# The rank product in three strips of the array, and a reordered work list around the batch boundaries of a fused attention and feed-forward kernel

## The chip, the cores and the metric

The kernel runs on one core of a Trainium2 chip. The metric is the device time of one execution in microseconds (us); lower is better. The profile comes from one further execution, whose own time is given below beside its span.

## The reference, cut to what matters

```python
B, H, S, D = 4, 8, 768, 48                     # 4 batches, 8 heads, 768 tokens, head size 48
f = 1 / (1 + exp(-f_logit))
for t in range(S):                             # gated linear attention
    state = f[:, :, t, :, None] * state + einsum('bhd,bhe->bhde', k[:, :, t], v[:, :, t])
    y[:, :, t] = einsum('bhd,bhde->bhe', q[:, :, t], state)
x = y as [B, S, 384]
u = x + ((x^T @ U) @ V)^T                      # token mix of rank 32: U is 768x32, V is 32x768
x2 = u + relu(u @ w_ch1) @ w_ch2               # 384 -> 1536 -> 384
h = relu(x2 @ w_in)                            # 384 -> 1024
c = conv along the tokens, 3 taps per channel
out = (h * sigmoid(c)) @ w_out                 # 1024 -> 384
```

## The kernel before, in words

The program is one list of tasks, `ORDER`, made by `schedule()` (line 69). Every engine walks through the same list and does its own share of each task; between engines there are only semaphores. So a change of the list changes what stands ahead of what on each engine.

**Attention.** A batch has 768 tokens, cut into 3 "duos" of 256 tokens, numbered n = 0 to 11 over the four batches. A duo goes through the steps of `STEPS`: EVEN (-1), levels 0 to 5, T (a transpose), U (state update), Y (outputs). In EVEN VectorE multiplies q by k for the self products (L1019) and q by the gates (L1022), GpSimd multiplies k by the gates (L1163) and then the gates in pairs (L1166). In a level TensorE forms scores with 32 small float32 matmuls in four quadrants of the array, 48 rows by 64 columns each (L585; level 0 has four wider ones ahead of them, L567), and VectorE scales q (L1029, L1040) and takes the scores out of PSUM (L976, L982). Y is L631, and ScalarE copies its result into `x` (L852, L853, L856; the last part of batch 0 on VectorE, L1063). The three duos of batch 0 run at the start with nothing else beside them. Those of batch b+1 run in slots of the feed-forward layers of batch b: `at` maps a slot s to attention steps.

**Layers of a batch.** `rank` forms x^T U: 6 float32 matmuls over the 6 token blocks, 128 rows by 96 columns (U three times side by side) by 384 (L668). ScalarE rounds it into `rstack` (L871) and VectorE writes the rest into rows 64 to 95 (L1070). `mix` transposes x and adds V times rank in the same PSUM bank (L679, L685), and u is split into u_hi and u_lo (ScalarE L876, VectorE L1077). `first1` and `second1` are the first layer pair, 24 slots: each product is made of three float32r matmuls from high and low parts (L700 to L702, L719, L720, L724), nine matmuls a task. `first2` and `second2` are the second pair, 16 slots (L739 to L741, L758, L759, L763). Between them ScalarE does the relu (L905), VectorE the convolution (L1109, L1112 twice), ScalarE the sigmoid (L892), VectorE the product (L1096), ScalarE the rounding (L898) and GpSimd the low part (L1200). `second2` of a task stands three slots after its `first2`. `out` copies three finished PSUM banks to `ostage` (ScalarE, L921).

**Weights.** 44 "pieces" of the weights are loaded during the first slots of batch 0, two per slot: SyncE issues the load, ScalarE rounds the high part (L863), GpSimd subtracts the low part (L1173), through 5 staging buffers.

**PSUM.** The ring `hb` of 3 banks serves rank, mix, first1 and first2 in turn (`ring_free` waits for the user three uses back); `acc` (3 banks) takes second1 and second2, `att` (2 banks) the attention.

**The order at the places in question, before.** Batch 0: Y of duo 1, rank of duo 0, Y of duo 2, rank of duos 1 and 2, pieces, mix 0 to 2, gates of duo 3, then slot 0 (first1, mix 3, EVEN of duo 3), slot 1 (first1, mix 4, 5, level 0 of duo 3), slot 2 (first1, level 1, second1). A batch's end: first2 15, second2 12, rank of the next batch, last2, second2 13, mix 0, mix 1, second2 14, mix 2, second2 15, out.

## Time and profile before

| | |
|---|---|
| median of 3 runs | 736.3 us (735.75 to 736.71) |
| profiled execution, own time | 736.56 us |
| its span, first to last instruction | 734.8 us |
| TensorE matmuls busy | 699.3 us, 95% |
| TensorE weight loads busy | 657.7 us, 90% |
| VectorE busy | 446.1 us, 61% |
| GpSimd busy | 286.3 us, 39% |
| ScalarE busy | 246.3 us, 34% |
| mean granted TensorE clock | 0.993 |

Times in the rows below count from the span's start. A float32 matmul is recorded as two matmul instructions, so the 6 matmuls of a rank are 12 records, and the 32 of an attention level are 64. In a timeline a merged row "x64" gives the start of the first and the time to the end of the last. The end of a matmul is modelled, so distances are read from start to start. The granted-clock column is a share of 2.4 GHz.

### The profile page before, as it was taken

The numbers are of one execution on the slowest core, as the hardware profiler recorded it, in microseconds if no ns is written. First come the engines' busy times: TensorE is split into PE (matmuls) and PEld (weight loads), VectorE is DVE, ScalarE is ACT, GpSimd is POOL, SyncE is SP. The second block draws the span as 40 slices with busy tenths as digits, with TensorE's granted clock in tenths as the row PEclk, the third lists the DMA queues.
The fourth block names the chain that finished last, engine by engine and source line by source line (L and its number), as shares of the span: only waits on it lengthen the run. The fifth ranks groups of instructions, "written<-read, shape, count | busy, mean of one in ns | idle before, by whom it ended". The sixth has DMA issues, their size and how long they took to land.

```text
span 734.8 us, 22489 instructions
## 1 busy us (share of the span) xinstructions
PE 699.3 (95%) x10076; PEld 657.7 (90%) x10076; DVE 446.1 (61%) x709; ACT 246.3 (34%) x504; POOL 286.3 (39%) x262
## 2 busy tenths in 40 slices
PE   2888799999999999999999999999999999999998
PEld 1777599989999889999999989999999889999997
DVE  6994565582798565365598755364489832121875
ACT  1134524333246432212245531313134542121453
POOL 5852567592363135043253224145145311030432
PEclk9999979999999999999999999999999999999999
DMA  8332353421101110200201200120000000000000
GB/s 202 102 89 52 82 141 106 118 73 47 43 1 55 45 54 7 62 24 24 67 2 27 72 34 24 25 65 23 24 2 2 34 33 1 0 1 1 1 33 32
DMA packets 24288, 33.67 MB, mean 46 GB/s; under 512 B 5152, under 2 KB 17184, under 8 KB 24192
## 3 DMA queue, kind: packets, MB, share of 16 engines
q1 hardware_dynamic: 23184, 30.46, 15.2%
q10 hardware_dynamic: 1008, 1.77, 1.1%
q8 instruction: 79, 1.29, 0.7%
q14 instruction: 17, 0.14, 0.1%
HBM read 27.50 MB, written 4.72 MB: 44 GB/s over the span
## 4 chain that ended last, share of the span: by engine, by line
PE 69%; DVE 21%; issue 5%; ACT 3%; DMA 1%; POOL 1%; ACTq 0%; DVEq 0%; POOLq 0%
PE acc L719 8%; PE hb L700 7%; PE acc L720 7%; PE acc L724 6%; PE hb L701 6%; PE hb L702 6%; PE att L585 5%; DVE conv L1112 5%; DVE q_t L1040 4%; PE att L631 3%; DVE conv L1109 3%; PE hb L668 2%; PE acc L758 2%; DVE conv L1096 2%; PE acc L759 2%
## 5 line engine op out<-in xcount | busy, mean ns | idle before, releaser
L1082 DVE SCALAR_TENSOR_TENSOR r_lo<-hb,r_hi 128x386 fp32r<-128x386 f32 (+1 forms) x96 | 53.4, 556 | 185.5 <-ACT r_hi L883 185.5
L883 ACT ACTIVATE r_hi<-hb 128x386 fp32r<-128x386 f32 (+1 forms) x96 | 47.2, 491 | 258.1 <-PE hb L702 258.1
L1200 POOL TENSOR_TENSOR r_lo<-conv,r_hi 128x384 fp32r<-128x384 f32 x64 | 61.8, 965 | 169.2 <-ACT r_hi L898 169.2
L1163 POOL TENSOR_TENSOR k_t<-k_t,blocks 112x512 f32<-112x512 f32 x60 | 82.5, 1376 | 83.3 <-PE att L585 72.3
L719 PE MATMUL acc<-r_hi,w_ch_hi 128*128 128x386 f32 (+1 forms) x288 | 103.7, 360 | 0.0
L700 PE MATMUL hb<-u_hi,w_ch_hi 128*128 128x386 f32 (+1 forms) x288 | 98.8, 343 | 3.0 <-DVE r_lo L1082 2.9
L701 PE MATMUL hb<-u_hi,w_ch_lo 128*128 128x386 f32 (+1 forms) x288 | 98.2, 341 | 0.0
L720 PE MATMUL acc<-r_hi,w_ch_lo 128*128 128x386 f32 (+1 forms) x288 | 97.9, 340 | 0.0
L702 PE MATMUL hb<-u_lo,w_ch_hi 128*128 128x386 f32 (+1 forms) x288 | 97.6, 339 | 0.0
L1112 DVE SCALAR_TENSOR_TENSOR conv<-hb,convw,conv 128x384 f32<-128x384 f32 x128 | 79.1, 618 | 4.5
L585 PEld LDWEIGHTS att<-q_t,k_t 48*64 48x64 f32 (+3 forms) x3840 | 60.0, 135 | 24.2 <-issue 17.6
L585 PE MATMUL att<-q_t,k_t 48*64 48x32 f32 (+3 forms) x3840 | 65.9, 220 | 9.1 <-DVE scores L976 4.0
L1040 DVE TENSOR_TENSOR q_t<-q_t,blocks 112x512 f32<-112x512 f32 x60 | 66.3, 1105 | 4.7 <-PE att L585 3.4
L758 PE MATMUL acc<-w_out_hi,r_hi 128*128 128x384 f32 x192 | 67.6, 352 | 1.3 <-ACT ostage L921 1.3
L724 PE MATMUL acc<-r_lo,w_ch_hi 128*128 128x386 f32 (+1 forms) x288 | 66.5, 339 | 0.0
L739 PE MATMUL hb<-u_hi,w_in_hi 128*128 128x388 f32 x192 | 65.4, 341 | 0.0
L741 PE MATMUL hb<-u_lo,w_in_hi 128*128 128x388 f32 x192 | 65.0, 338 | 0.0
L740 PE MATMUL hb<-u_hi,w_in_lo 128*128 128x388 f32 x192 | 64.8, 338 | 0.0
L759 PE MATMUL acc<-w_out_lo,r_hi 128*128 128x384 f32 x192 | 64.6, 337 | 0.0
L1163 POOL TENSOR_TENSOR k_t<-k_t,gates 112x512 f32<-112x512 f32 x12 | 18.5, 1542 | 113.6 <-DVE blocks L1019 108.7
L700 PEld LDWEIGHTS hb<-u_hi,w_ch_hi 128*128 128x128 f32 x288 | 54.9, 191 | 3.9 <-DVE r_lo L1082 3.3
L719 PEld LDWEIGHTS acc<-r_hi,w_ch_hi 128*128 128x128 f32 x288 | 54.6, 189 | 2.3
(138 smaller groups left out, 1313.5 us busy)
## 6 DMA issues: line engine op xcount, KB each, us to landing
v_p<-in_vn_dram SPq DMA_DIRECT2D x12, 384.0 KB, 3.9
out_dram<-ostage SPq DMA_DIRECT2D x24, 192.0 KB, 2.1
q_t<-in_qT_dram SPq DMA_DIRECT2D x21, 192.0 KB, 3.4
k_t<-in_kT_dram SPq DMA_DIRECT2D x21, 192.0 KB, 3.3
gates<-in_fT_dram SPq DMA_DIRECT2D x21, 192.0 KB, 3.5
ostage<-in_w_ch_dram SPq DMA_DIRECT2D x14, 192.0 KB, 3.3
conv<-in_w_ch_dram SPq DMA_DIRECT2D x10, 192.0 KB, 3.0
ostage<-in_w_out_dram SPq DMA_DIRECT2D x5, 192.0 KB, 2.8
```

What stands on the lines that cost most here:

```text
L585: mm = pe.matmul(banks[o:o + left, par, g * C + half:g * C + half + 32], k[rows, first:first + left], moving, start=True, stop=True, skip_ ...
L700: pe.matmul(o, wh[:, t, ws], u_hi[:, t, cols], start=(t == 0), stop=False)
L701: pe.matmul(o, wl[:, t, ws], u_hi[:, t, cols], start=False, stop=False)
L702: mm = pe.matmul(o, wh[:, t, ws], u_lo[:, t, cols], start=False, stop=(t == CT - 1))
L719: pe.matmul(o, wh[:, j, ws], r_hi[:, s, 0:width], start=(j == 0), stop=False)
L720: pe.matmul(o, wl[:, j, ws], r_hi[:, s, 0:width], start=False, stop=False)
L724: mm = pe.matmul(o, wh[:, j, ws], r_lo[:, s, 0:width], start=False, stop=(j == N1 - 1))
L758: pe.matmul(o, r_hi[:, s, ts], wh[:, j, :], start=(j == 0), stop=False)
L759: pe.matmul(o, r_hi[:, s, ts], wl[:, j, :], start=False, stop=False)
L1040: nc.vector.tensor_tensor(view, view, block_product(products(gates[i], blocks[i], st), c, 0), ALU.mult).then_inc(q_ready, 1)
L1112: nc.vector.scalar_tensor_tensor(out=c, in0=hid[:, tap + 1:HALF + tap + 1], scalar=convw[:, j, tap:tap + 1], in1=c, op0=ALU.mult, op1=ALU. ...
L1163: nc.gpsimd.tensor_tensor(view, view, block_product(ends, c, 1), ALU.mult).then_inc(k_ready, 1)
```

## The change

1. `rank`: U is kept once (`mixu` 32 columns wide). The six matmuls are 128 rows by 32 columns and go to three strips of 32 PSUM partitions in turn (block t to strip t % 3). VectorE adds the three strips into `rank_sum` (a copy and two additions); a new task `rank_split` lets ScalarE write three rounded copies of 32 rows (rows 64 to 95 first) and VectorE subtract for the low part. `mix` waits for all of them.
2. Batch 0: EVEN and gates of duo 3 go ahead of Y of duos 1 and 2, all rank work behind both Y, level 0 of duo 3 ahead of the mix; all later attention steps of batch 0's layers come two slots earlier.
3. A batch's end: rank of the next batch ahead of second2 12, then the last gate, `rank_split`, last2, second2 13, 14, mix 0 to 2, second2 15.
4. GpSimd's first product of a duo (k by the gates) waits until VectorE's q product has ended, not only for the self products and the gates.
5. The rounding and low part of the second pair's tasks (`split2`) move to the end of the slot, behind `out`, attention copies and x2 splits; the states task goes ahead of first2.
6. The constants of the mix take 6 DMAs in place of 8.

```diff
-        if st == Y and n > 0:
-            order.append(("rank", 0, n - 1))
         if n == DUOS - 1 and st == U:
+            order += [("gates", DUOS), ("att", DUOS, EVEN)]
             order += [("piece", i) for i in range(FIRST)]
     for b in range(B):
         if b == 0:
-            order += [("rank", 0, DUOS - 1)] + [("piece", FIRST + i) for i in range(3)]
-            order += [("mix", 0, i) for i in range(CT)] + [("gates", DUOS)]
+            order += [("rank", 0, j) for j in range(DUOS)] + [("rank_split", 0), ("att", DUOS, 0)]
+            order += [("piece", FIRST + i) for i in range(3)] + [("mix", 0, i) for i in range(CT)]
...
+                    if b == 0:
+                        s -= 2
+                        if s < 0:
+                            continue
...
             else:
+                order += [("states", n) for n, st in at.get(s - 1, []) if st == U]
                 order.append(("first2", b, s - 2 * N1))
-            order += [("states", n) for n, st in at.get(s - 1, []) if st == U]
+            if s < 2 * N1:
+                order += [("states", n) for n, st in at.get(s - 1, []) if st == U]
...
+            if b + 1 < B and s == 2 * N1 + 2 * N2 - 1:
+                order += [("rank", b + 1, j) for j in range(DUOS)]
             if q >= 0:
                 order.append(("second2", b, q))
                 if q % N2 == N2 - 1:
                     order.append(("out", b, q // N2))
+            if s > 2 * N1:
+                order.append(("split2", b, s - 2 * N1 - 1))
         more = b + 1 < B
-        order += [("rank", b + 1, j) for j in range(DUOS)] * more + [("last2", b), ("second2", b, 2 * N2 - 3)]
-        order += [("mix", b + 1, i) for i in range(2)] * more + [("second2", b, 2 * N2 - 2)]
-        order += [("mix", b + 1, 2)] * more + [("second2", b, 2 * N2 - 1), ("out", b, 1)]
+        order += [("last_gate", b)] + [("rank_split", b + 1)] * more + [("last2", b)]
+        order += [("second2", b, 2 * N2 - 3), ("second2", b, 2 * N2 - 2)]
+        order += [("mix", b + 1, i) for i in range(CT)] * more + [("second2", b, 2 * N2 - 1), ("out", b, 1)]
...
                 for t in range(2 * j, 2 * j + 2):
-                    pe.matmul(ring_bank(use, DM)[0:3 * RANK, :], mixu[:, t, :], x[:, t, :],
-                              start=(t == 0), stop=(t == UNITS - 1)).then_inc(rank_done, 1)
+                    g = slice(RANK * (t % 3), RANK * (t % 3) + RANK)
+                    pe.matmul(ring_bank(use, DM)[g, :], mixu[:, t, :], x[:, t, :], start=(t < 3), stop=(t >= 3),
+                              skip_group_check=True).then_inc(rank_done, 1)
...
                 if i == 0:
                     pe.wait_ge(rank_ready, b + 1)
+                    pe.wait_ge(rank_hi_ready, 3 * (b + 1))
...
-            def rank_task(b, j):
-                if j < DUOS - 1:
-                    return
-                act.wait_ge(rank_done, UNITS * (b + 1))
+            def rank_split(b):
+                act.wait_ge(rank_summed, 3 * (b + 1))
                 if b > 0:
                     act.wait_ge(mix_done, 2 * CT * b)
-                nc.scalar.copy(rstack[:], ring_bank(ring_use(b, "rank", 0), DM)[0:3 * RANK, :]).then_inc(rank_hi_ready, 1)
+                for i in (2, 0, 1):
+                    nc.scalar.copy(rstack[RANK * i:RANK * (i + 1), :], rank_sum[:]).then_inc(rank_hi_ready, 1)
...
-                if q >= 1:
-                    cast2(b, q - 1)
...
+                elif kind == "last_gate":
+                    sigmoid2(task[1], 2 * N2 - 1)
+                elif kind == "split2":
+                    cast2(*task[1:])
                 elif kind == "last2":
-                    sigmoid2(task[1], 2 * N2 - 1)
                     cast2(task[1], 2 * N2 - 1)
...
-                dve.wait_ge(rank_hi_ready, b + 1)
+                dve.wait_ge(rank_done, UNITS * (b + 1))
...
+                sums = [ring_bank(ring_use(b, "rank", 0), DM)[RANK * i:RANK * (i + 1), :] for i in range(3)]
+                nc.vector.tensor_copy(rank_sum[:], sums[0]).then_inc(rank_summed, 1)
+                for i in (1, 2):
+                    dve.wait_ge(rank_summed, 3 * b + i)
+                    nc.vector.tensor_tensor(rank_sum[:], sums[i], rank_sum[:], ALU.add).then_inc(rank_summed, 1)
+
+            def rank_split(b):
+                dve.wait_ge(rank_hi_ready, 3 * b + 1)
                 lo = slice(2 * RANK, 3 * RANK)
-                nc.vector.tensor_tensor(rstack[lo, :], ring_bank(ring_use(b, "rank", 0), DM)[lo, :], rstack[lo, :],
-                                        ALU.subtract).then_inc(rank_ready, 1)
+                nc.vector.tensor_tensor(rstack[lo, :], rank_sum[:], rstack[lo, :], ALU.subtract).then_inc(rank_ready, 1)
...
                 if st == 0:
-                    pool.wait_ge(selves_ready, selves(n))
-                    pool.wait_ge(gates_ready, n + 1)
+
+                    pool.wait_ge(q_ready, scaled(n, EVEN))
...
-                elif kind == "first2" and task[2] >= 1:
-                    lo2(task[1], task[2] - 1)
+                elif kind == "split2":
+                    lo2(*task[1:])
```

## Rows read from the trace of the kernel before

**Rows 1.** The page, part 1: busy us, share of the span, instructions.
```profile
PE 699.3 (95%) x10076; PEld 657.7 (90%) x10076; DVE 446.1 (61%) x709; ACT 246.3 (34%) x504; POOL 286.3 (39%) x262
```
**Rows 2.** Windows: stretch, busy us by engine, granted clock, DMA share, GB/s.
```profile
25.00:35.00 10.00, 8.58 (x304) 7.81 (x304) 9.89 (x12) 0.00 (x0) 8.79 (x7) 1.00 0.69 181
...
90.80:92.00 1.20, 0.00 (x0) 0.00 (x0) 1.20 (x3) 0.00 (x0) 1.20 (x2) 0.52 0.82 190
92.00:97.00 5.00, 4.96 (x73) 4.52 (x73) 3.67 (x5) 1.30 (x3) 1.34 (x2) 0.50 0.94 242
97.00:101.00 4.00, 4.00 (x20) 3.94 (x17) 1.92 (x2) 0.00 (x0) 3.72 (x4) 0.50 0.15 34
```
**Rows 3.** Timeline, batch 0's rank: start us, us, engine line op.
```profile
71.41 2.69 PE L668 MATMUL hb<-x,mixu 128*96 128x384 f32 x4
...
74.03 1.15 PE L631 MATMUL hb<-state,q_t 48*64 48x48 f32 x64
...
76.35 2.82 PE L668 MATMUL hb<-x,mixu 128*96 128x384 f32 x8
...
79.20 0.47 ACT L871 CAST rstack<-hb 96x384 fp32r<-96x384 f32 x1 [1.74 <-PE hb L668]
...
80.32 0.45 PE L685 MATMUL hb<-vstack,rstack 96*128 96x386 f32 x1 [0.72 <-DVE rstack L1070]
```
**Rows 4.** Timeline, slots 1 and 2 of batch 0; in brackets idle before, releaser.
```profile
86.60 4.92 DVE L1022 TENSOR_TENSOR q_t<-q_t,gates 112x512 f32<-112x512 f32 x1
...
87.00 0.66 PE L567 MATMUL att<-blocks,ones 48*64 48x256 f32 x8
...
88.13 1.14 PE L585 MATMUL att<-q_t,k_t 48*64 48x32 f32 x64 [0.47 <-POOL k_t L1163]
...
92.05 0.69 PE L700 MATMUL hb<-u_hi,w_ch_hi 128*128 128x386 f32 x1 [2.78 <-DVE r_lo L1082]
...
95.25 1.93 PE L585 MATMUL att<-q_t,k_t 48*64 48x32 f32 x64
```
**Rows 5.** Timeline, the end of batch 0 and the start of batch 1.
```profile
250.09 1.27 DVE L1112 SCALAR_TENSOR_TENSOR conv<-hb,convw,conv 128x384 f32<-128x384 f32 x2
250.21 4.03 PE L668 MATMUL hb<-x,mixu 128*96 128x384 f32 x12
...
254.65 0.53 ACT L892 ACTIVATE conv<-conv 128x384 f32<-128x384 f32 x1
...
256.55 1.01 POOL L1200 TENSOR_TENSOR r_lo<-conv,r_hi 128x384 fp32r<-128x384 f32 x1 [5.73 <-ACT r_hi L898]
...
258.47 0.60 PE L679 MATMUL hb<-ident_r,x 128*128 128x128 f32 x4
...
259.08 0.34 PE L758 MATMUL acc<-w_out_hi,r_hi 128*128 128x384 f32 x1
...
260.66 0.34 PE L700 MATMUL hb<-u_hi,w_ch_hi 128*128 128x386 f32 x1
```
**Rows 6.** Timeline, products of VectorE and GpSimd in the start phase.
```profile
10.95 0.69 DVE L1022 TENSOR_TENSOR q_t<-q_t,gates 112x512 f32<-112x512 f32 x1 [0.80 <-ACT gates L805]
...
17.67 2.02 DVE L1022 TENSOR_TENSOR q_t<-q_t,gates 112x512 f32<-112x512 f32 x1
...
32.65 1.09 POOL L1163 TENSOR_TENSOR k_t<-k_t,blocks 112x512 f32<-112x512 f32 x1
```
**Rows 7.** Timeline, ScalarE and TensorE at the first `out` of batch 0.
```profile
231.47 1.24 ACT L921 COPY ostage<-acc 128x384 f32<-128x384 f32 x3
...
232.10 0.41 PE L758 MATMUL acc<-w_out_hi,r_hi 128*128 128x384 f32 x1 [0.34 <-ACT ostage L921]
```
**Rows 8.** Timeline, two further stalls of TensorE at attention levels.
```profile
154.43 3.81 DVE L1040 TENSOR_TENSOR q_t<-q_t,blocks 112x512 f32<-112x512 f32 x1
...
159.02 0.92 PE L585 MATMUL att<-q_t,k_t 48*48 48x32 f32 x64 [1.30 <-DVE scores L982]
...
270.08 1.14 PE L585 MATMUL att<-q_t,k_t 48*64 48x32 f32 x64 [0.94 <-DVE scores L976]
```

More of the change, by code:

```diff
@@ L314, in bass_gla_lowrank_mix_ffn_gated_conv_ffn @@
         wsplit = {"ch1": weight("ch1", [P, CT, FF1]), "ch2": weight("ch2", [P, N1, DM])}
-        mixu = sb("mixu", [P, UNITS, 3 * RANK])
+        mixu = sb("mixu", [P, UNITS, RANK])
+        rank_sum = sb("rank_sum", [RANK, DM])
         vstack = sb("vstack", [3 * RANK, S], F32R)
@@ L385, in bass_gla_lowrank_mix_ffn_gated_conv_ffn @@
         x_copied, x_copied_last = sem("x_copied"), sem("x_copied_last")
-        rank_done, rank_hi_ready, rank_ready = sem("rank_done"), sem("rank_hi_ready"), sem("rank_ready")
+        rank_done, rank_summed = sem("rank_done"), sem("rank_summed")
+        rank_hi_ready, rank_ready = sem("rank_hi_ready"), sem("rank_ready")
         mix_done, u_hi_ready, u_lo_ready = sem("mix_done"), sem("u_hi_ready"), sem("u_lo_ready")
@@ L476, in consts_mix @@
             def consts_mix():
+                sp.dma_start(mixu[:], mix_u.rearrange("(t p) r -> p t r", p=P)).then_inc(loaded_mix, 16)
                 for i in range(3):
-                    sp.dma_start(mixu[:, :, RANK * i:RANK * (i + 1)],
-                                 mix_u.rearrange("(t p) r -> p t r", p=P)).then_inc(loaded_mix, 16)
                     sp.dma_start(x[RANK * i:RANK * (i + 1), 2:4, :].rearrange("r a b -> r (a b)"), mix_v).then_inc(
@@ L664, in rank_task @@
                 if j == 0:
-                    pe.wait_ge(loaded_mix, 96)
+                    pe.wait_ge(loaded_mix, 64)
                     ring_free(use)
                 for t in range(2 * j, 2 * j + 2):
-                    pe.matmul(ring_bank(use, DM)[0:3 * RANK, :], mixu[:, t, :], x[:, t, :],
-                              start=(t == 0), stop=(t == UNITS - 1)).then_inc(rank_done, 1)
+                    g = slice(RANK * (t % 3), RANK * (t % 3) + RANK)
+                    pe.matmul(ring_bank(use, DM)[g, :], mixu[:, t, :], x[:, t, :], start=(t < 3), stop=(t >= 3),
+                              skip_group_check=True).then_inc(rank_done, 1)
             def mix_task(b, i):
@@ L833, in attention @@
                     if n == 0:
-                        act.wait_ge(loaded_mix, 96)
+                        act.wait_ge(loaded_mix, 64)
                         nc.scalar.copy(vstack[:], x[0:3 * RANK, 2:4, :].rearrange("r a b -> r (a b)")).then_inc(vstack_hi, 1)
@@ L932, in _ @@
                     piece(task[1])
-                elif kind == "rank":
-                    rank_task(*task[1:])
+                elif kind == "rank_split":
+                    rank_split(*task[1:])
                 elif kind == "mix":
@@ L1067, in rank_task @@
                     return
-                dve.wait_ge(rank_hi_ready, b + 1)
+                dve.wait_ge(rank_done, UNITS * (b + 1))
+                if b > 0:
+                    dve.wait_ge(rank_ready, b)
+                    dve.wait_ge(rank_hi_ready, 3 * b)
+                sums = [ring_bank(ring_use(b, "rank", 0), DM)[RANK * i:RANK * (i + 1), :] for i in range(3)]
[5 more added lines that the diff above has]
+                dve.wait_ge(rank_hi_ready, 3 * b + 1)
                 lo = slice(2 * RANK, 3 * RANK)
-                nc.vector.tensor_tensor(rstack[lo, :], ring_bank(ring_use(b, "rank", 0), DM)[lo, :], rstack[lo, :],
-                                        ALU.subtract).then_inc(rank_ready, 1)
+                nc.vector.tensor_tensor(rstack[lo, :], rank_sum[:], rstack[lo, :], ALU.subtract).then_inc(rank_ready, 1)
             def mix_task(b, i):
@@ L1123, in _ @@
                     rank_task(*task[1:])
+                elif kind == "rank_split":
+                    rank_split(*task[1:])
                 elif kind == "mix":
```

## The prediction

> **What bounds the kernel now.** I read the page's busy shares first, then the same in windows, then the waits, then the timeline where TensorE pauses. TensorE is busy 95% of the span, no other engine over 61% [rows 1]. So a change pays in three ways only: less TensorE work, fewer of its pauses, or fewer microseconds at the lower clock. The start phase is different: there VectorE is full (9.89 of 10 us) and TensorE waits for it between small matmuls [rows 2].
>
> The clock needs care. The column says 1.00 in the start phase, but 4 records of the rank took 2.69 us at 71.41 and 8 took 2.82 us at 76.35 [rows 3]: the first lot ran at half the rate, 1.2 GHz. An attention level of 64 records takes 1.14 us at 88.13 and 1.93 us at 95.25, where the column says 0.50 [rows 2, 4]. So the core starts at 1.2 GHz, is at 2.4 from about 74, drops to 1.2 in the pause ahead of 92.05 and is back after 101 [rows 2, 4].
>
> **1. The strips.** A rank costs TensorE 12 x 0.322 = 3.87 us at the full clock (12 records, 4.03 us with the last one's tail) [rows 5]. Three strips can at best run together: 4 x 0.322 = 1.3 us. At worst they follow one another: 3.87 us. The nearest row is level 0's L567: 8 records of 256 columns in four quadrants took 0.66 us [rows 4]; in a row they would be 8 x 0.215 (two thirds of 0.322) = 1.72 us. That is an overlap of 2.6 with four tiles, some 2.4 with three, so 1.6 us: 2.25 saved per rank. Full-height strips are no quadrants, therefore both ends stay in the range.
>
> The Trainium skill ("TensorE: Matmul & The Clock Gate", Part 3, the table of measured speedups) gives 2.38 times for three column tiles of 32; with it a rank would be 1.63 us. No row here shows that shape.
>
> At the ends of batches 0, 1 and 2 TensorE has no pause around the rank, so the saving counts in full if the longer chain behind it stays covered: 3 x 2.25 = **6.75**. The chain: the rank now begins one second2 (1.58 us, 259.08 to 260.66) earlier, near 248.6, and VectorE has task 15's convolution to do until 251.4 [rows 5], 2.8 us after that. Then its copy and two additions, 0.64 us each as L1112's PSUM reads (1.27 for two), ScalarE's first copy 0.5 (L871, rows 3), the subtraction 0.6: rank_ready some 5.9 us after the rank's start, and ScalarE's third copy 0.2 later. TensorE has 1.6 (rank) + 3 x 1.58 (second2 12 to 14) = 6.3 us of work before the first mix. Task 15's product stands behind the sum on VectorE, then cast and low part, which end about 8 us after the start; second2 15 needs the low part only in its last third, at 6.3 + 3 x 0.61 (a mix, 258.47 to 259.08) + 1.0 = 9.2 us. Covered, by 0.2 to 0.4 and by 1.2 us. Without that cover each us of lateness costs one us. In the old order the sigmoid of task 15 came at 254.65 and its low part at 256.55 [rows 5], so this end had been waiting for the rank too.
>
> The skill's "TensorEngine Tiling (Array Packing)" (PSUM Bottleneck) warns that reading PSUM out may become the limit once the array is faster. By that rule the gain per end would be what the cover leaves, 2.25 while it holds. It holds here by the sum above.
>
> **2. The start of the layers in batch 0.** Three gains. (a) The pause of 2.78 us ahead of 92.05 goes [rows 4]: VectorE's L1022 took 4.92 us there, beside GpSimd, whose weight pieces it shared the stretch with, and r_lo and u_lo waited behind it. After the change EVEN of duo 3 stands where VectorE and GpSimd idle, behind the last state update. (b) Level 0 of duo 3 (86.99 to 89.27, 2.3 us with its wait) moves under the wait for the rank's sum. (c) From 92.05 to 101 TensorE was dense at 1.2 GHz: 9 us for 4.5 us of work [rows 2]. Sum 9.6 us. Against it: the rank's chain from last matmul to ready is now 3.3 us where it was 1.15 (79.17 to 80.32) [rows 3], balanced by the six matmuls' 1.6 us where 2.69 and 2.82 stood; VectorE takes level 0's scores ahead of u_lo, 0.3 us late; the weight pieces 0 to 2 come on GpSimd some 3.5 us later, behind duo 3's k product, still ahead of first1 0; in slot 2 level 3 follows level 2 by one first1 of 1.58 us, shorter than VectorE's q product and scores, 0.4 us. SyncE gets duo 4's q load ahead of pieces (no wait in it) and its gates load two slots earlier (waits for level 0, which is done). That leaves 8 us if the clock rises as early as before.
>
> I doubt that. It rose during dense 128-row matmuls of the rank at 71.41 to 74 [rows 3], while the attention before it, with TensorE 8.58 of 10 us busy, had not raised it [rows 2], and at 95.25 an attention level stood in the stretch that stayed at 0.50 [rows 2, 4]. After the change attention outputs of duo 2, narrow strips and level 0 come first, and dense work begins only with the mix near 82. Then Y of duo 2, rank, level 0, the mixes and most of first1 0 (8.6 us at full clock: 2.4, 1.6, 1.8, 1.8 and 1.0) take twice that. The chains of VectorE and ScalarE between them run at their own speed and hide about half of the 8.6, so +4.2 us, leaving 3.8. I take **4.5**, ends 3 and 8.
>
> **3. k behind q.** With GpSimd beside it L1022 takes 2.02 us, alone 0.69; GpSimd's product alone is 1.09 [rows 6]. So q is ready 1.3 us earlier, k about 0.3 us later (0.69 + 1.09 against the 1.5 from 86.60 to TensorE's start at 88.13, rows 4). In the start phase VectorE is full, which would give 1.3 us for each of duos 1 and 2; but then GpSimd, 8.79 of 10 us busy [rows 2], ends its chain later and gives most of it back. I take **0.7**, ends -0.5 and 1.8. At the starts of batches 1 and 2 level 1 waited 0.94 us for the scores behind L1022 [rows 8]; 0.4 us of each goes: **0.8**.
>
> **4. Output copies first.** At the first `out` of a batch second2 8 waited 0.34 us for copies (0.41 us each, 1.24 for three) that stood behind a rounding on ScalarE [rows 7]. Without it they start a rounding earlier, about one such copy, and the wait goes, in three batches: **1.0**, ends 0 and 1.5. In batch 3 the same move delays task 9's low part; the gate loop catches up by the end, 0.2 at most, left at nothing. The rounding at a slot's end is used a full slot later: covered by TensorE's 3.1 us slot.
>
> **5. The shift by two slots.** The stall of 1.30 us ahead of 159.02 comes from an L1040 that took 3.81 us beside GpSimd's pieces and splits [rows 8]. Levels meet the pieces elsewhere now: I take **0.6**, ends -1 and 1.3. Two DMAs fewer lie at 30 us, where nobody waits for them: nothing.
>
> **Sum:** 6.75 + 4.5 + 0.7 + 0.8 + 1.0 + 0.6 = 14.35. From the profiled execution's 736.56 us that is 722.2; the median of the runs is 0.3 lower, so **722**.
>
> **Rivals.**
> - *The clock rises early* (0.16): the first dense pieces are enough. For it: the rise before came within 3 us of rank work. Gain of part 2 is 8: 718.5, down to 716 with the upper ends.
> - *The strips don't overlap* (0.15): each float32 matmul has two passes and its own increment, and they run in a row. For it: no row shows three full-height strips. Then the 6.75 goes, and batch 0's wait grows a little: 729.
> - *Weight pieces are late* (0.08): pieces start 3.5 us later on GpSimd and TensorE reaches first1 3 and second1 1 some 6 us sooner. By my walk through the list piece 8 is split near 90 and needed at 94 to 100. If GpSimd is slower, TensorE waits 4 to 6 us in slots 2 to 8: 727.
> - *The lower clock stays* (slower, 0.04): attention in every slot keeps TensorE at 1.2 GHz. Everything but the clock gains about 19 us (9.85 elsewhere, 5 in pause and level 0, 4.5 of the old slow stretch). A us of dense time at half rate costs half a us, so it must last from 74 to about 112 to undo all, and to 118 it gives 739. Against it: before, it rose at 101 amid such slots.
> - *Nothing measurable* (0.02): several of these together.
>
> The forecast itself has 0.55, its own range 718.5 to 726. The range 716 to 729.5 takes in the first three rivals. A measurement here tells about 0.2% (1.5 us) from no change. Faster 0.94, within it 0.02, slower 0.04.
>
> **What the profile after would show.** The rank: 12 records in about 1.6 us at the three batch ends, no pause ahead of the first mix or second2 15. L1022 at 0.7 us in most duos. No pause of over 1 us between 84 and 100. The column of the clock: a rise after 80 for the forecast, at 74 for the first rival, a second drop for the fourth. TensorE's first copy-bound wait at second2 8 gone. I'm wrong if the rank takes over 3 us, if a pause appears ahead of first1 3 to 8, or if the start phase up to Y of duo 1 has become longer by over 1 us.

## The result, and the profile after

The changed kernel took 725.27 us (median of 4 runs, 722.35 to 728.22), the kernel before 736.02 us on the same chip (735.29 to 736.71): ratio 0.9854, 95% interval [0.9813, 0.9895], so 10.7 us less. The profiled execution took 722.35 us, the fastest of the four, with a span of 720.5 us. The same kernel a second time, on another chip, gave 726.0 us (the kernel before on that chip: 735.3) and a ratio of 0.9862 [0.9841, 0.9882]. I had said 722.0, range 716 to 729.5.

The page's part 1 after, to be held against [rows 1]: 16.2 us less of busy TensorE, 16.0 us less of VectorE.

```profile
PE 683.1 (95%) x10076; PEld 644.5 (89%) x10076; DVE 430.1 (60%) x721; ACT 251.0 (35%) x512; POOL 282.6 (39%) x262
```

**Where the time went.** The first `first1` matmul of each batch is a milestone that both traces have. Timeline of before (the start of batch 1, 260.66, stands in [rows 5]):

```profile
82.03 0.41 PE L700 MATMUL hb<-u_hi,w_ch_hi 128*128 128x386 f32 x1
...
431.70 0.34 PE L700 MATMUL hb<-u_hi,w_ch_hi 128*128 128x386 f32 x1
...
602.58 0.34 PE L700 MATMUL hb<-u_hi,w_ch_hi 128*128 128x386 f32 x1
```

And of after:

```profile
80.23 0.52 PE L712 MATMUL hb<-u_hi,w_ch_hi 128*128 128x386 f32 x1
...
249.69 0.34 PE L712 MATMUL hb<-u_hi,w_ch_hi 128*128 128x386 f32 x1
...
419.06 0.34 PE L712 MATMUL hb<-u_hi,w_ch_hi 128*128 128x386 f32 x1
...
588.32 0.34 PE L712 MATMUL hb<-u_hi,w_ch_hi 128*128 128x386 f32 x1
```

The differences of these starts, with the same ones of the experiments (each kernel's own profiled execution, us):

| kernel | start of batch 0's layers | batch 0 | batch 1 | batch 2 |
|---|---|---|---|---|
| before | 82.0 | 178.6 | 171.0 | 170.9 |
| after | 80.2 | 169.5 | 169.4 | 169.3 |
| after, again | 84.4 | 169.1 | 169.4 | 169.3 |
| rank_wide | 84.6 | 173.0 | 171.6 | 171.5 |
| strip_pairs | 81.0 | 172.0 | 169.4 | 169.3 |
| k_old | 84.4 | 171.2 | 167.8 | 167.7 |
| k_hybrid | 81.8 | 171.2 | 167.8 | 167.6 |
| no_shift | 84.1 | 175.3 | 169.3 | 169.3 |
| split_old | 80.2 | 169.1 | 170.2 | 169.9 |
| loose | 82.2 | 164.8 | 166.8 | 166.7 |

Batch 3 takes 128.2 us to its last matmul in before and after alike. So the 14.2 us between the two profiled executions are 1.8 up to the start of the layers, 9.2 in batch 0, 1.7 in batch 1 and 1.6 in batch 2. The last two columns repeat within 0.1 to 0.3 us wherever the code is the same; the first column does not (80.2 and 84.4 for the same kernel). Small terms are therefore read from the last two.

The column of batch 0 carries the clock with it. After and its variants had between none and 10.3 us at 0.50 around the start of the layers, and a dense microsecond at half rate costs half a microsecond. Batch 0 of after_again had none and took 169.1. Rank_wide had 3.4 us of it: 169.1 + 2.2 (wide rank, below) + 1.7 is its 173.0. In strip_pairs 6.4 us of it fall in batch 0: 169.1 + 3.2 is 0.3 over its 172.0. In k_old and k_hybrid it is 6.8 us: their 171.2 hides that they are shorter at the full clock, by about 1.3.

**The rank.** Timeline of after at the end of batch 0, to be held against [rows 5]:

```profile
240.02 1.49 PE L679 MATMUL hb<-x,mixu 128*32 128x384 f32 x12
...
242.55 0.54 DVE L1085 COPY rank_sum<-hb 32x384 f32<-32x384 f32 x1
...
243.12 1.14 DVE L1088 TENSOR_TENSOR rank_sum<-hb,rank_sum 32x384 f32<-32x384 f32 x2
...
244.29 1.59 ACT L882 CAST rstack<-rank_sum 32x384 fp32r<-32x384 f32 x3 [1.10 <-DVE rank_sum L1088]
...
244.83 0.55 DVE L1093 TENSOR_TENSOR rstack<-rank_sum,rstack 32x384 fp32r<-32x384 f32 x1 [0.57 <-ACT rstack L882]
...
246.59 1.00 POOL L1224 TENSOR_TENSOR r_lo<-conv,r_hi 128x384 fp32r<-128x384 f32 x1 [4.34 <-ACT r_hi L909]
246.63 0.42 PE L697 MATMUL hb<-vstack,rstack 96*128 96x386 f32 x1
...
248.13 0.34 PE L770 MATMUL acc<-w_out_hi,r_hi 128*128 128x384 f32 x1
```

Twelve records in 1.49 us where they took 4.03. The chain behind them ends at 245.38 (subtraction) and 245.88 (third copy). The first product that needs it starts at 246.63 with no bracket, and so does second2 15 at 248.13. The longer chain is hidden, with 0.75 us to spare.

**Batch 0's slot 2.** The pause of 2.78 us that the change was to remove [rows 4] is gone, and another has come. Timeline of after:

```profile
87.91 3.12 DVE L1052 TENSOR_TENSOR q_t<-q_t,blocks 112x512 f32<-112x512 f32 x1
...
88.38 1.15 POOL L1187 TENSOR_TENSOR k_t<-k_t,blocks 112x512 f32<-112x512 f32 x1
...
89.49 2.40 POOL L1197 TENSOR_TENSOR w_ch_lo<-conv,w_ch_hi 128x384 fp32r<-128x384 f32 x2
...
90.96 0.69 DVE L994 COPY_PREDICATED scores<-masks,att 128x512 f32<-128x512 uint8 x1
91.80 1.03 PE L595 MATMUL att<-q_t,k_t 48*56 48x32 f32 x64 [2.18 <-DVE scores L994]
```

VectorE's q product, 0.69 us when nothing holds it up, takes 3.12 beside GpSimd's work: a low part of a weight piece that was already running, the k product, and two further low parts. Behind it stand level 2's scores, and TensorE waits 2.18 us for these ahead of level 3.

**The clock.** Windows of after (columns as in [rows 2]):

```profile
74.00:77.40 3.40, 2.00 (x76) 1.60 (x73) 2.73 (x5) 1.59 (x4) 0.05 (x1) 1.00 0.91 222
77.40:80.80 3.40, 3.38 (x13) 3.25 (x14) 2.60 (x4) 2.58 (x6) 2.87 (x3) 0.50 0.26 69
...
84.00:101.00 17.00, 14.82 (x318) 13.66 (x318) 12.81 (x17) 5.63 (x13) 14.86 (x13) 1.00 0.51 137
```

One stretch of 3.4 us at 0.50, against 10.2 us before. The fall follows the wait for the sum, 1.42 us ahead of the first L697. That wait alone doesn't settle it: the second execution of after had it too (1.46 us) and no fall.

### The profile page after: what moved, and what is told of

It reads as the page before. It is cut to its first block, busy times and chain, and to the rows that moved or that the text cites. A ratio compares the mean times of both kernels' runs of the same rounds, so it can differ in the third digit from the quotient of the medians.

```text
span 720.5 us, 22499 instructions
## 1 busy us (share of the span) xinstructions
PE 683.1 (95%) x10076; PEld 644.5 (89%) x10076; DVE 430.1 (60%) x721; ACT 251.0 (35%) x512; POOL 282.6 (39%) x262
## 4 chain that ended last, share of the span: by engine, by line
PE 86%; DVE 5%; POOL 4%; issue 3%; ACT 2%; DMA 1%; ACTq 0%; DVEq 0%; POOLq 0%
PE acc L731 8%; PE att L595 8%; PE acc L732 7%; PE acc L736 6%; PE hb L712 6%; PE hb L713 6%; PE hb L714 6%; PE acc L770 5%; PE hb L751 5%; PE hb L753 5%; PE hb L752 5%; PE acc L771 5%; PE acc L775 5%; PE att L641 3%; POOL k_t L1187 3%
## 5 line engine op out<-in xcount | busy, mean ns | idle before, releaser
L1224 POOL TENSOR_TENSOR r_lo<-conv,r_hi 128x384 fp32r<-128x384 f32 x64 | 63.7, 995 | 147.3 <-ACT r_hi L909 147.3
L1187 POOL TENSOR_TENSOR k_t<-k_t,blocks 112x512 f32<-112x512 f32 x60 | 81.7, 1364 | 89.9 <-PE att L595 81.0
L595 PEld LDWEIGHTS att<-q_t,k_t 48*64 48x64 f32 (+3 forms) x3840 | 58.7, 134 | 28.9 <-issue 16.8
L1052 DVE TENSOR_TENSOR q_t<-q_t,blocks 112x512 f32<-112x512 f32 x60 | 60.1, 1002 | 4.1 <-PE att L595 2.4
L903 ACT ACTIVATE conv<-conv 128x384 f32<-128x384 f32 x64 | 33.7, 526 | 77.1 <-DVE conv L1134 77.1
```

Of the source, the lines that this page charges most:

```text
L595: mm = pe.matmul(banks[o:o + left, par, g * C + half:g * C + half + 32], k[rows, first:first + left], moving, start=True, stop=True, skip_ ...
L1187: nc.gpsimd.tensor_tensor(view, view, block_product(ends, c, 1), ALU.mult).then_inc(k_ready, 1)
```

## The experiments

Results with their ratio to the kernel before on the same chips. Differences of medians below are partly between chips and so good to about 1 us. Edits are against the changed kernel unless stated.

| run | median us (lowest to highest) | ratio, 95% |
|---|---|---|
| rank_wide | 734.1 (729.82 to 735.11) | 0.9966 [0.9944, 0.9988] |
| strip_pairs | 726.96 (725.64 to 728.28) | 0.9878 [0.9848, 0.9908] |
| k_old | 723.9 (722.57 to 725.04) | 0.9853 [0.9833, 0.9874] |
| k_hybrid | 722.05 (719.17 to 722.42) | 0.9816 [0.9791, 0.9841] |
| no_shift | 730.32 (728.3 to 732.02) | 0.9935 [0.9908, 0.9962] |
| split_old | 726.38 (723.41 to 727.02) | 0.9873 [0.9855, 0.9891] |
| after_again | 726.0 (724.11 to 726.91) | 0.9862 [0.9841, 0.9882] |
| loose | 714.62 (712.6 to 715.04) | 0.9705 [0.9685, 0.9724] |
| warm2 | 726.55 (725.88 to 727.2) | 0.9877 [0.9853, 0.9901] |
| warm4 | 735.88 (717.27 to 737.38) | none |
| warm_late | 716.13 (714.48 to 717.33) | 0.9734 [0.9712, 0.9757] |

**rank_wide: the strips undone, everything else kept.**

```diff
-                    g = slice(RANK * (t % 3), RANK * (t % 3) + RANK)
-                    pe.matmul(ring_bank(use, DM)[g, :], mixu[:, t, :], x[:, t, :], start=(t < 3), stop=(t >= 3),
+                    pe.matmul(ring_bank(use, DM)[0:3 * RANK, :], mixu[:, t, :], x[:, t, :],
+                              start=(t == 0), stop=(t == UNITS - 1)).then_inc(rank_done, 1)
...
```

The rest of the edit makes `mixu` 96 columns wide again and puts one ScalarE copy and one subtraction in place of the sums and the three copies.

> The changed kernel with the rank as before (96 columns wide, accumulated over all six blocks, one ScalarE copy and one subtraction), everything else as changed. If the strips' overlap is the gain at the batch ends, each rank is 3.87 us again and each end 2.3 us longer: 7 us slower from three ends and 0 to 2 us in batch 0, where the shorter split chain gives some back. Rival: the gain at the ends comes from the rank's earlier place, since the sigmoid of task 15 no longer waits; then the ends grow by under 1 us each.

Its timeline at the end of batch 0:

```profile
245.61 4.03 PE L678 MATMUL hb<-x,mixu 128*96 128x384 f32 x12
249.68 0.47 ACT L879 CAST rstack<-hb 96x384 fp32r<-96x384 f32 x1 [0.81 <-PE hb L678]
```

Batches 1 and 2 take 2.2 us more each than after's, in exchange for a shorter chain behind the rank, which was hidden. That is the strips' whole worth in a steady batch, and the 2.25 of the sum. So the rival (ends longer by under 1 us each) is out. Over the whole kernel the medians differ by 8.1 to 8.8 us for four ranks, three of which the sum counted at 6.75. The profiled executions say where: against after_again 2.2 in each of batches 1 and 2, 3.9 in batch 0 (the wide rank at its end and 3.4 us at the lower clock) and 0.2 ahead of it.

**strip_pairs: blocks 0 and 1 to strip 0, 2 and 3 to strip 1, 4 and 5 to strip 2.**

```diff
-                    g = slice(RANK * (t % 3), RANK * (t % 3) + RANK)
-                    pe.matmul(ring_bank(use, DM)[g, :], mixu[:, t, :], x[:, t, :], start=(t < 3), stop=(t >= 3),
+                    g = slice(RANK * (t // 2), RANK * (t // 2) + RANK)
+                    pe.matmul(ring_bank(use, DM)[g, :], mixu[:, t, :], x[:, t, :], start=(t % 2 == 0), stop=(t % 2 == 1),
```

> The changed kernel with blocks 0 and 1 on strip 0, 2 and 3 on strip 1, 4 and 5 on strip 2, so that two matmuls in a row share a strip. If TensorE starts work in order and overlap needs the next record to be on another strip, the 12 records take 2.6 to 3.2 us in place of 1.5 and each batch end is 1.1 to 1.7 us longer (whole: 4 to 6 us). If work of a strip is queued by itself and order doesn't matter, 1.5 us as before.

The rank of batch 1 in this kernel's timeline:

```profile
243.34 1.50 PE L679 MATMUL hb<-x,mixu 128*32 128x384 f32 x12
```

1.50 against 1.49 us, batches 1 and 2 as in after. Neighbours in program order need not lie in different strips for the strips to overlap.

**k_old: GpSimd's first k product does not wait for q (part 4 undone). k_hybrid: it waits in the start phase only.** The edit shown is k_hybrid's; k_old has the two old waits for every duo.

```diff
-                if st == 0:
+                if st == 0 and n < DUOS:
                     pool.wait_ge(q_ready, scaled(n, EVEN))
+                elif st == 0:
+                    pool.wait_ge(selves_ready, selves(n))
+                    pool.wait_ge(gates_ready, n + 1)
```

> The changed kernel with part 4 undone: GpSimd's first product of a duo waits only for the self products and the gates. Theory A: that product takes 1.5 us with or without VectorE beside it, so waiting for q only makes k 0.7 us later, and level 0 of each of the nine duos in the layers stalls TensorE for it. Then the batch period (first1 0 of batch 1 to that of batch 2, 169.4 us in the changed kernel) falls by 1.2 to 2 us and the whole by 3 to 5 us. Theory B, the one of the prediction: q early is worth more than k late; the period grows by 0.4 and the whole by 1 to 2 us.

> The changed kernel with part 4 kept for the three duos of the start phase and undone for the nine in the layers. Theory A: as k_old in the layers (period 1.2 to 2 us shorter) and within 1 us of the changed kernel up to the first outputs, so 3 to 5 us faster in all. It tells what k behind q is worth in the start phase, where VectorE is full: duo 1's Y starts at 65.0 us in the changed kernel; if k_old starts it at 66 to 67, the gain at the start is of part 4. Theory B: slower by 1 us.

This is where the sum had the wrong sign. Timeline of after at the start of batch 1 (EVEN, level 0, level 1 of the first duo):

```profile
253.76 0.69 DVE L1034 TENSOR_TENSOR q_t<-q_t,gates 112x512 f32<-112x512 f32 x1
254.53 1.50 POOL L1187 TENSOR_TENSOR k_t<-k_t,gates 112x512 f32<-112x512 f32 x1 [6.94 <-DVE q_t L1034]
256.08 1.14 PE L595 MATMUL att<-q_t,k_t 48*64 48x32 f32 x64 [0.93 <-POOL k_t L1187]
...
259.41 1.14 PE L595 MATMUL att<-q_t,k_t 48*64 48x32 f32 x64 [0.39 <-DVE scores L988]
```

And of k_old, the same instructions:

```profile
259.64 1.51 POOL L1187 TENSOR_TENSOR k_t<-k_t,gates 112x512 f32<-112x512 f32 x1 [6.14 <-DVE blocks L1031]
259.67 2.03 DVE L1034 TENSOR_TENSOR q_t<-q_t,gates 112x512 f32<-112x512 f32 x1
261.20 1.13 PE L595 MATMUL att<-q_t,k_t 48*64 48x32 f32 x64
...
265.05 1.14 PE L595 MATMUL att<-q_t,k_t 48*64 48x32 f32 x64 [0.93 <-DVE scores L988]
```

The q product does fall from 2.03 to 0.69. But the k product takes 1.50 us in both traces, so it ends 0.7 to 0.8 us later, and TensorE waits for k ahead of level 0 (0.93). Level 1's wait shrinks from 0.93 to 0.39. For the first duo that is 0.39 more than before (0.93 + 0.39 against 0.93), and the second and third duos, where nothing waited, now wait about 0.4 us each (row of the second duo of batch 1 in after: below; the third's is 0.42). These waits make 1.2 us. By the milestones the whole costs 1.6 us a batch, 169.4 against 167.8; the last 0.4 stands in no bracket.

```profile
302.23 1.14 PE L595 MATMUL att<-q_t,k_t 48*64 48x32 f32 x64 [0.39 <-POOL k_t L1187]
```

By the medians the whole kernel gained 1.4 us in k_old and 3.2 in k_hybrid, where I had expected 3 to 5 of both; k_old missed it.

Why 1.50 in both? Both traces have a k product that was never held up. Where the two products start together, the one that starts second waits, and in the rows above that was VectorE's, by 0.03 us. k_old also has the other case, at the EVEN of duo 3:

```profile
71.41 0.69 DVE L1034 TENSOR_TENSOR q_t<-q_t,gates 112x512 f32<-112x512 f32 x1
71.44 2.03 POOL L1187 TENSOR_TENSOR k_t<-k_t,gates 112x512 f32<-112x512 f32 x1 [10.89 <-DVE blocks L1031]
```

Here VectorE's came 0.03 us first: it takes 0.69 and GpSimd's 2.03. Whoever is first, both are done 2.06 us after the first start. With the wait they run one behind the other and take 2.27 (after, 253.76 to 256.03). So the wait makes q early and k late, and level 0 needs k.

In the start phase the profiles don't resolve the wait: Y of duo 0 starts at 58.0 to 60.1 us in seven kernels with the wait, at 59.4 and 60.1 in the two without it (before and k_old). The runs say more. k_hybrid differs from k_old in this alone, on the same chip, and each of its five runs (719.2 to 722.4) is below the lowest of k_old's (722.6 to 725.0): 1.9 us less by the medians. In the two profiled executions the layers start at 81.8 and 84.4; 2.1 of the 2.6 us are there at the first Y (58.0 against 60.1). One profile of each can't tell the wait's share of that from the spread.

**no_shift: batch 0's attention in the old places.** EVEN, gates and level 0 of duo 3 back in the slots, no shift by two.

```diff
-            order += [("gates", DUOS), ("att", DUOS, EVEN)]
...
-            order += [("rank", 0, j) for j in range(DUOS)] + [("rank_split", 0), ("att", DUOS, 0)]
-            order += [("piece", FIRST + i) for i in range(3)] + [("mix", 0, i) for i in range(CT)]
+            order += [("rank", 0, j) for j in range(DUOS)] + [("rank_split", 0)]
+            order += [("piece", FIRST + i) for i in range(3)] + [("mix", 0, i) for i in range(CT)] + [("gates", DUOS)]
...
-                    if b == 0:
-                        s -= 2
-                        if s < 0:
-                            continue
```

> The changed kernel with batch 0's order of attention as before: EVEN and gates of duo 3 in slot 0, level 0 in slot 1, no shift by two slots; strips and the place of the rank stay changed. If the shift made the gain of batch 0 (first1 0 to batch 1's first1 0: 178.7 us before, 169.5 after), the stall of 2 to 3 us behind level 0 is back with a stretch at half the clock, and batch 0 is 5 to 7 us longer. Rival: the order of the rank alone removed it (rank work no longer between the outputs); then under 2 us longer.

4.3 to 5.0 us slower than after by the medians. In its profile batch 0 takes 175.3 us against 169.5 and 169.1. The stall behind level 0 is back, smaller than expected:

```profile
96.88 1.26 PE L590 MATMUL att<-q_t,k_t 48*64 48x32 f32 x64 [1.86 <-DVE scores L983]
```

Windows of no_shift:

```profile
80.70:87.50 6.80, 6.17 (x23) 5.95 (x24) 1.73 (x4) 5.29 (x12) 4.12 (x5) 0.50 0.34 89
...
97.70:101.20 3.50, 3.50 (x33) 3.44 (x26) 1.91 (x2) 0.00 (x0) 2.96 (x3) 0.51 1.06 244
```

10.3 us at the lower clock; the second execution of after had none. Batch 0's layers start at 84.1, so 6.9 of the 10.3 fall in batch 0, and at most 3.4 us of its 5.8 to 6.2 can be the clock. The other 2.4 us at least are the order: level 0 of duo 3, 1.8 us of TensorE, now stands among the layers, while ahead of them the wait for the rank's sum grew from 1.42 and 1.46 us to 2.96. Whether the order also causes the lower clock, this one profile can't say.

**split_old: rounding of the second pair back ahead of the output copies (part 5 undone).**

```diff
                 order.append(("first2", b, s - 2 * N1))
+                if s > 2 * N1:
+                    order.append(("split2", b, s - 2 * N1 - 1))
...
-            if s > 2 * N1:
-                order.append(("split2", b, s - 2 * N1 - 1))
```

> The changed kernel with part 5 undone: rounding and low part of a gated task again right behind first2, ahead of attention copies, x2 splits and output copies. If that order made the gain at second2 8, the pauses of 0.7 to 0.9 us there are back in batches 1 and 2 (period 169.4 becomes 170.0 to 170.3) and the whole is 1 to 2 us longer. If the gain came from elsewhere, no change of the period.

Its timeline at the first `out` of batch 1, the wait of [rows 7] back again:

```profile
392.77 1.25 ACT L930 COPY ostage<-acc 128x384 f32<-128x384 f32 x3
393.40 0.41 PE L770 MATMUL acc<-w_out_hi,r_hi 128*128 128x384 f32 x1 [0.52 <-ACT ostage L930]
```

Batches 1 and 2 take 0.8 and 0.6 us more; batch 0 takes 0.4 less than in after and the same as in after_again. The whole run, 726.38 against 725.27 and 726.0, can't show it.

**after_again: the changed kernel a second time.**

> The changed kernel once more, for its spread (722.35 to 728.22 in four runs). If the spread is the clock's, the runs fall in the same 6 us again, and the profile shows the start phase at half clock until 74 or later and a pause-and-drop pair near 82 to 100, where the first profile had its rise at 60. If the profile looks like the first, its time is near 722.

Its batches repeat; its layers start at 84.4 instead of 80.2. Of these 4.2 us 1.4 are there when the first Y starts (58.7 and 60.1). The reason for the rest stands in Y of duos 0 and 2, attention products of 64 records each. In after (two timeline rows; the column of the clock says 1.00 at all four rows shown here):

```profile
60.64 1.15 PE L641 MATMUL att<-v_p,scores 64*64 64x48 f32 x64
...
68.24 1.14 PE L641 MATMUL hb<-state,q_t 48*64 48x48 f32 x62
```

In the second execution:

```profile
62.32 1.96 PE L641 MATMUL att<-v_p,scores 64*64 64x48 f32 x64
...
71.92 1.92 PE L641 MATMUL hb<-state,q_t 48*64 48x48 f32 x64
```

1.14 or 1.15 us against 1.92 to 1.96 for the same work: at 60.6 the one was already at 2.4 GHz, the other still at 1.2 at 72 and until about 78. Over the profiles this rise came at 60 (after, split_old, strip_pairs), at 72 to 75 (loose, k_hybrid, before) or at 77 to 78 (after_again, k_old, rank_wide, no_shift), and the layers started at 80.2 to 81.0, 81.8 to 82.2, and 84.1 to 84.6. Counted from the first Y the layers start 21.5 to 22.3 us later with the rise at 60, 22.6 to 23.8 with it at 72 to 75, and 24.3 to 25.3 with it at 77 to 78. In the two executions of after this makes 2.8 of the 4.2 us. The pause-and-drop pair that I had expected near 82 to 100 came as a pause alone, 2.19 us ahead of 95.63.

One more pause is new. After_again at the first `first1`:

```profile
84.39 0.41 PE L712 MATMUL hb<-u_hi,w_ch_hi 128*128 128x386 f32 x1 [0.86 <-POOL w_ch_lo L1197]
```

A weight piece's low part is late there. The same wait stands in every variant but no_shift, 0.86 to 0.99 us long; in the first execution of after and in no_shift the mixes ran at the lower clock (1.17 us from one to the next, against 0.61), and the low part was done 1.3 us before first1 0. Before had no such wait.

**loose: more room between what depends on each other.** On k_hybrid: batch 0's duo 3 has level 3 and later one slot later than in the change (so no level stands in slot 2), and in batches 1 and 2 levels 1 and later of the first duo come one slot later.

```diff
-                        s -= 2
+                        s -= 1 if j == 0 and s >= 4 else 2
                         if s < 0:
                             continue
+                    elif j == 0 and i >= 2:
+                        s += 1
```

> k_hybrid with no attention level in slot 2, where the slot has one first1 only: in batch 0 duo 3's level 3 and later steps come one slot later (shift by one in place of two), in batches 1 and 2 the first duo's levels from 1 on. Theory: the pause of 2.5 us ahead of level 3 in batch 0 (near 94.6 in k_hybrid), the drop of the clock behind it (3.4 us at half, 1.7 us) and the pauses of 1.27 us in batches 1 and 2 come from VectorE having one first1 (1.6 us) between two levels; they go, and the whole is 5 to 6 us under k_hybrid, near 717. Rival: the starved VectorE product moves with the level and stalls TensorE one slot later; then under 1.5 us.

714.62 us, ratio 0.9705: faster than both kernels, 10.7 us ahead of the changed one (11.4 of its runs on the same chip) and 7.4 ahead of k_hybrid, more than the 5 to 6 I had expected. VectorE's slow product is still there. Timeline of loose around the same place:

```profile
89.52 3.13 DVE L1054 TENSOR_TENSOR q_t<-q_t,blocks 112x512 f32<-112x512 f32 x1
...
92.58 0.72 DVE L996 COPY_PREDICATED scores<-masks,att 128x512 f32<-128x512 uint8 x1
...
94.32 1.03 PE L597 MATMUL att<-q_t,k_t 48*56 48x32 f32 x64
...
254.99 1.30 DVE L990 COPY_PREDICATED scores<-first_mask,att 128x1024 f32<-128x1024 uint8 x1
...
258.66 1.14 PE L597 MATMUL att<-q_t,k_t 48*64 48x32 f32 x64
```

3.13 us as before, but level 3 comes 1.0 us after the scores instead of waiting for them, and no bracket stands there nor at level 1 of batch 1 (258.66). The window 84 to 101 is full: 17.00 us of TensorE in 17, at the full clock.

```profile
84.00:101.00 17.00, 17.00 (x331) 15.90 (x329) 13.06 (x17) 8.10 (x18) 15.69 (x16) 1.00 0.65 178
```

Against k_hybrid batch 0 gains 6.4 us, batches 1 and 2 gain 1.0 and 0.9 (their wait of 0.93 at level 1). Of the 6.4, 2.2 is a pause like after's at 91.80 and 0.6 one ahead of 120.78; k_hybrid also had 6.8 us at the lower clock (81.7 to 85.1 and 95.4 to 98.8) and loose none, up to 3.4 more.

**warm2, warm4, warm_late: does extra dense work raise the clock early?** On loose, matmuls of 128x128 by 512 columns into a PSUM bank that is free at that time, whose result nothing reads: 2 or 4 ahead of every attention step of the start phase but EVEN, and 4 ahead of the first mix; in warm_late 4 ahead of T, U and Y of duo 2 and of the first mix alone.

```diff
+            still = ident_r[:].rearrange("p (o m) -> p o m", o=1).broadcast_to([P, 4, P])
+
+            def keep_busy(count):
+                for _ in range(count):
+                    pe.matmul(acc[:, 2, :].rearrange("p (o m) -> p o m", m=P), ident_r[:], still, start=True, stop=True,
+                              skip_group_check=True)
...
             def attention(n, st):
+                if n < DUOS and st != EVEN:
+                    if (n, st) == (0, 0):
+                        pe.wait_ge(padded, 5)
+                    keep_busy(2)
...
+                    if task[1:] == (0, 0):
+                        keep_busy(4)
```

> The kernel loose with two extra matmuls (128 rows by 128 columns by 512, identity times itself, into an unused PSUM bank, result never read) ahead of each attention step of the start phase and four ahead of the first mix. If the lower clock of the start costs time, the clock rises well before 60 us, attention levels take 1.1 us in place of 1.9 and first1 0 starts 3 to 6 us earlier than loose's 82.2; the whole is 709 to 712 us. If VectorE alone sets the start phase, the first outputs come at the same time as in loose and only the part from 65 us on gains, 1 to 2 us. If the extra work costs more than the clock gives, it is slower.

> As warm2 with four extra matmuls ahead of each step. At half clock they take 1.7 us a step, at full clock 0.9. If two are too few to raise the clock, four do, and the start phase is shorter than in warm2; if two were enough, four cost 0 to 5 us more, since TensorE then has more work in the start phase than it had pauses.

> The kernel loose with four extra matmuls ahead of T, U and Y of duo 2 and ahead of the first mix only. It tells whether the clock's state at the first outputs and the rank, where the forecast saw +4.2 us, sets the time: the rise then comes by 62 to 66 instead of 72 to 78, first1 0 starts at 80 to 81 in place of 82 to 84, and the spread of the runs falls under 2 us. Rival: the spread is of the DMA or of the start phase before 60 us and stays.

Not as I thought. Windows and a timeline row of warm2, the start phase:

```profile
25.00:35.00 10.00, 10.00 (x226) 7.50 (x226) 7.93 (x11) 0.00 (x0) 6.53 (x5) 1.00 0.37 114
```

```profile
55.52 1.22 PE L564 MATMUL acc<-ident_r 128*128 128x512 f32 x2
...
60.29 0.73 PE L564 MATMUL acc<-ident_r 128*128 128x512 f32 x2
...
72.71 1.13 PE L654 MATMUL att<-state,q_t 48*64 48x48 f32 x48
```

TensorE was busy 10 of 10 us and stayed at 1.2 GHz all the same: the two added matmuls of a step, which take 0.73 us at 60.29, still took 1.22 at 55.52, and the starts of each pair before that lie 0.59 us apart, against 0.34 from 60.29 on. The rise came at 60, as in three kernels without them. Meanwhile Y of duo 0 slid from 59 to 72.7 us, because at 1.2 GHz the added work had made TensorE the bound. warm4 pushed it to 84.2, and four of its five runs took 731.9 to 737.4, one 717.3; its profiled execution is of the long kind. In warm4 the rise came between 67.5 and 69.7, the latest added matmul at half rate and the first at full. Warm_late tells less than it was meant to: Y of duo 0 already ran at the full clock at 61.45 (64 records in 1.15 us), and its first added matmul starts at 62.52, so the added work didn't cause its rise. Its layers started at 82.2 like loose's, and its runs spread over 2.9 us, not under 2. The 16 added matmuls may have taken what the early rise gave; that isn't shown.

## Why the prediction was right or wrong, by its own steps

**1. The strips (6.75 forecast).** Right in mechanism and size: a rank of 1.49 us where 1.6 was taken from the overlap of level 0, and 2.2 us a batch against rank_wide. The cover held: 5.4 and 5.9 us for the chain where 5.9 and 6.1 were worked out. The rival that they don't overlap is excluded by the row at 240.02. The Trainium skill ("TensorE: Matmul & The Clock Gate", Part 3) gives 2.38 times for three column tiles; here 4.03 us became 1.49, tails counted in both, which is 2.7 times.

**2. Start of the layers in batch 0 (4.5 forecast).** Near in size with the wrong account. No_shift undoes most of this part together with part 6: 4.3 to 5.0 us where 5.1 were forecast for the two. The working was loose: the gains less the losses that I gave a number leave 8.9 us, not 8, and I took 4.5 where they then gave 3.8. The old pause of 2.78 went, and I had allowed 0.4 us for level 3 close behind level 2; it cost 2.18. The step that failed: the 0.4 came from VectorE's q product and scores at their undisturbed length, though [rows 4] and [rows 8] showed 4.92 and 3.81 us beside GpSimd, and the shift put exactly such a product under the weight pieces. The criterion "no pause of over 1 us between 84 and 100" caught it. Another term failed too: the weight pieces were to come "still ahead of first1 0", and one is 0.86 us late in after_again. The clock made up for it: 3.4 us or none at the lower clock in the profiled executions of after, where 10.2 had stood, which neither the forecast (a rise after 80) nor its rival (74) had. It rose at 60 or at 78, and the same kernel did both.

**3. k behind q in the start phase (0.7 forecast).** The right way: k_hybrid is 1.9 us under k_old, near the forecast's upper end. How much of this the wait itself gives isn't shown; the profiles don't resolve it.

**4. k behind q in the layers (0.8 gain forecast).** Wrong in sign: 1.6 us lost in each of batches 1 and 2, 3.2 together, a miss of 4.0 us by itself. The step that failed: "GpSimd's product alone is 1.09", "k about 0.3 us later". The 1.09 of [rows 6] is one product by `blocks`; the first product of a duo is by `gates`, and takes 1.50 us when it isn't held up. With the wait it starts, and ends, 0.7 to 0.8 us later. The "alone 0.69" was misread too: at 10.95 GpSimd's k product stood beside VectorE's from 11.09 on and took 1.89 us. VectorE's was short because it came first. Only the waits at level 1 had been looked at [rows 8]; that level 0 waits for k was written into [rows 4] (0.47 <-POOL k_t) and was left out. Batch 0 has the loss as well, about 1.3 us by k_old's 171.2 once its lower clock is taken off.

**5. Output copies first (1.0 forecast).** Right mechanism: the wait is gone. Undersized per batch: 0.7 in each of batches 1 and 2, where 0.34 was taken from the bracket alone, and nothing in batch 0.

**6. The shift by two slots (0.6 forecast).** The stall of 1.30 us ahead of 159.02 is not in after's trace and is back in no_shift, 1.28 us ahead of 160.16. It is part of no_shift's 4.3 to 5.0.

**Sum.** In steady batches: strips 2.2 and output copies 0.7 gained, k 1.6 lost, so 1.3 of the 1.6 us measured per batch. 3 x 2.2 + 2 x 0.7 - 2 x 1.6 = 4.8; with no_shift's 4.3 to 5.0 that is 9.1 to 9.8, where the medians show 10.7 (9.3 in after_again). The agreement is rough: batch 0's loss by part 4 and part 3 are left out, and no_shift's figure holds the clock. So the forecast gain of 14.35 was 3.6 too high, and step 4 alone explains 4.0. That the profiled execution met 722 to 0.4 us is chance: it was the fastest, with the early rise.

**The rivals.** The early rise (718.5) has its clock in some executions and not its time. The late weight pieces (727): they came twice, smaller than the rival had it. Through VectorE's product they made the pause of 2.2 us ahead of level 3, and as late data one of 0.86 us ahead of first1 0 in after_again, not 4 to 6 us in slots 2 to 8. The lower clock to the end: 3.4 us at most.

**Still open:** what raises the clock at 60, 73 or 78 us, since TensorE at 10 of 10 us did not; whether the order of the work in no_shift causes its lower clock; and what the wait for q gives in the start phase.

## What to carry to other kernels

Price an operation by a row of the same operands and form: GpSimd's product by `gates` takes 1.50 us, while one by `blocks` took 1.09, and the 60 of that form in before's trace run from 1.05 to 1.84. One row is not a price until it's clear what stood beside it, and which of the two began first. When an order is tightened, look at which instruction sits beside a shared resource in its new place and at its longest row, not at its undisturbed one; a slot of distance between a result and its user was worth 7.4 us here (loose against k_hybrid, up to 3.4 of them the clock), about as much as the strips (8.1 to 8.8). And read small terms from a stage that repeats to 0.1 us, not from whole runs that differ by 3 to 6.

## What the runs showed of the hardware

- Three strips of 32 columns with all 128 rows run together: 12 records in 1.49 us against 4.03 for one tile 96 columns wide, and in 1.50 when neighbours share a strip.
- VectorE's q product and GpSimd's k product, both 112x512 from SBUF, hold each other up, and the one that starts second pays. With GpSimd 0.02 to 0.03 us ahead they take 1.50 and VectorE's 2.03 (k_old, 259.64); with VectorE 0.03 us ahead 0.69 and GpSimd's 2.03 (k_old, 71.41). Behind a train of GpSimd work VectorE's took 3.12 (after, 87.91) and 4.92 (before, 86.60).
- The core's clock rose from 1.2 to 2.4 GHz at 60 to 61, 68 to 70, 72 to 75 or 77 to 78 us of the profiled executions, with the granted-clock column at 1.00 all the time; only the length of known work (64 records in 1.14 or 1.92 us) shows it. For one and the same kernel the rise at 60 rather than 78 was worth 2.8 us between the first Y and the layers.
